# The last chunk's products with w_out as two products of 256 columns each

## The reference, cut to what matters

```
def _moe2_ref(x, w_in, w_out, s, b):
    h = x @ w_in                 # 4608 x 512 @ 512 x 2048
    r = np.maximum(h, 0.0)
    g = s * (r * r) + b
    return (g @ w_out)           # 4608 x 2048 @ 2048 x 512
```

## Time and profile before

| What | us |
| --- | --- |
| median of 3 runs | 681.55 (679.55 to 682.57) |
| the profiled execution's own time | 681.13 |
| its span, first to last instruction | 679.3 |
| PE busy over the span | 646.2 (95%) |
| stretch of the last chunk's products, about 628.0 to 674.7 | 46.7 |

### The profile page before, as it was taken

The page is one execution under the profiler, slowest core; times in us unless marked ns, Lnnn a source line. Parts: engine busy times, 40 slices in busy tenths (PEclk is TensorE's granted clock), DMA queues, the critical chain, the costliest instruction groups (busy, mean ns, idle before and its releaser), DMA issues.

```text
span 679.3 us, 13164 instructions
## 1 busy us (share of the span) xinstructions
PE 646.2 (95%) x5170; PEld 501.3 (74%) x5170; DVE 369.3 (54%) x610; ACT 325.4 (48%) x599; POOL 114.8 (17%) x117
## 2 busy tenths in 40 slices
PE   6787999989998889999999999999999999999997
PEld 6565677767653248888888888888888888888885
DVE  5757575646344747664454454554544554545543
ACT  1576777767421165654344444443444434443442
POOL 3799777622210000000000000000000000000000
PEclk8899999989999999999999999999999999999999
DMA  9688959573489930010010010000000100100101
GB/s 339 223 264 301 357 201 404 172 295 127 156 311 429 425 166 1 1 52 11 1 62 1 1 62 0 25 37 0 31 31 0 62 0 0 62 1 0 63 0 63
DMA packets 25233, 80.45 MB, mean 118 GB/s; under 512 B 6496, under 2 KB 14688, under 8 KB 22368
## 3 DMA queue, kind: packets, MB, share of 16 engines
q1 hardware_dynamic: 25184, 79.76, 31.5%
HBM read 70.32 MB, written 9.44 MB: 117 GB/s over the span
## 4 chain that ended last, share of the span: by engine, by line
PE 83%; DMA 8%; POOL 3%; DVE 2%; issue 2%; ACT 1%; ACTq 0%; SPq 0%; DVEq 0%; POOLq 0%
PE bank L1467 19%; PE bank L1469 19%; PE bank L1468 19%; PE bank L1451 5%; DMA late<-in_moe_w_dram 4%; PE bank L1318 4%; DMA kvbuf<-in_k_dram 3%; PE bank L1305 2%; PE bank L1242 2%; PE bank L1275 2%; PE bank L1401 2%; PE bank L1348 2%; POOL kvbuf L664 1%; PE bank L1364 1%; PE bank L1201 1%
## 5 line engine op out<-in xcount | busy, mean ns | idle before, releaser
L1467 PE MATMUL bank<-w_hi,r_hi 128*128 128x512 f32 x576 | 224.4, 389 | 1.4 <-DVE r_lo L1099 1.4
L1468 PE MATMUL bank<-w_lo,r_hi 128*128 128x512 f32 x576 | 224.2, 389 | 0.0
L1469 PE MATMUL bank<-w_hi,r_lo 128*128 128x512 f32 x576 | 224.2, 389 | 0.0
L1093 DVE SCALAR_TENSOR_TENSOR win_sb<-win_sb,sb_col 128x512 f32<-128x512 f32 x144 | 108.4, 753 | 197.6 <-ACT win_sb L845 197.5
L845 ACT ACTIVATE win_sb<-bank 128x512 f32<-128x512 f32 x144 | 86.2, 598 | 217.7 <-PE bank L1451 217.7
L1467 PEld LDWEIGHTS bank<-w_hi,r_hi 128*128 128x128 f32 x576 | 108.1, 188 | 24.4 <-DVE r_lo L1099 2.0
L1469 PEld LDWEIGHTS bank<-w_hi,r_lo 128*128 128x128 f32 x576 | 108.1, 188 | 22.4
L1468 PEld LDWEIGHTS bank<-w_lo,r_hi 128*128 128x128 f32 x576 | 108.1, 188 | 22.4
L1099 DVE SCALAR_TENSOR_TENSOR r_lo<-win_sb,sb_col,r_hi 128x512 fp32r<-128x512 f32 x144 | 107.6, 747 | 1.5 <-ACT r_hi L854 1.5
L854 ACT ACTIVATE r_hi<-win_sb,sb_col 128x512 fp32r<-128x512 f32 x144 | 103.3, 717 | 1.6 <-PE bank L1469 1.6
L1451 PE MATMUL bank<-cT,g_st 128*128 (+1 forms) x144 | 56.4, 393 | 0.0
(11 more groups left out here) (131 smaller groups left out, 552.3 us busy)
## 6 DMA issues: line engine op xcount, KB each, us to landing
early_third<-in_moe_w_dram SPq DMA_DIRECT2D x6, 2048.0 KB, 14.1
kvbuf<-in_k_dram SPq DMA_DIRECT2D x12, 768.0 KB, 5.5
kvbuf<-in_v_dram SPq DMA_DIRECT2D x12, 768.0 KB, 6.2
out_dram<-win_sb SPq DMA_DIRECT2D x36, 256.0 KB, 2.4
qbuf<-in_q_dram SPq DMA_DIRECT2D x8, 1024.0 KB, 9.1
early<-in_moe_w_dram SPq DMA_DIRECT2D x4, 2048.0 KB, 12.4
late<-in_moe_w_dram SPq DMA_DIRECT2D x4, 2048.0 KB, 20.2
win_sb<-in_moe_w_in_dram SPq DMA_DIRECT2D x4, 1024.0 KB, 5.3
```

Of the source, the lines that this page charges most:

```text
L1093: dve.scalar_tensor_tensor(out=g_sb[:, n % 2, :], in0=r_sb[:, n % 2, :], scalar=sb_col[:, 0:1], in1=r_sb[:, n % 2, :], op0=ALU.mult, op1=A ...
L1467: pe.matmul(acc, r2_hi[:, f % 2, toks], w_hi[:, f, :], start=(f == 0), stop=False)
L1468: pe.matmul(acc, r2_hi[:, f % 2, toks], w_lo[:, f, :], start=False, stop=False)
L1469: last = pe.matmul(acc, r2_lo[:, f % 2, toks], w_hi[:, f, :], start=False, stop=(f == F2C - 1))
```

## The change: what it does

In chunk 8 each product with `w_out` becomes two: the loop over `cols` makes the three products for columns 0 to 255 of the bank and then the three for columns 256 to 511. The weights are loaded anew for each. The flag `start`, which makes a product overwrite instead of add, is set on the first product of the bank alone (f = 0, left half). The two semaphore increments stay on the last product of their m. Chunks 0 to 7 have one part of 512 columns as before.

```
-                        acc = acc_bank(odd, m)[:, :]
-                        pe.matmul(acc, r2_hi[:, f % 2, toks], w_hi[:, f, :], start=(f == 0), stop=False)
-                        pe.matmul(acc, r2_hi[:, f % 2, toks], w_lo[:, f, :], start=False, stop=False)
-                        last = pe.matmul(acc, r2_lo[:, f % 2, toks], w_hi[:, f, :], start=False, stop=(f == F2C - 1))
+                        acc = acc_bank(odd, m)
+                        cols = (slice(0, D // 2), slice(D // 2, D)) if final else (slice(0, D),)
+                        for x, part in enumerate(cols):
+
+                            first_part = f == 0 and x == 0
+                            pe.matmul(acc[:, part], r2_hi[:, f % 2, toks], w_hi[:, f, part], start=first_part, stop=False,
+                                      skip_group_check=True)
+                            pe.matmul(acc[:, part], r2_hi[:, f % 2, toks], w_lo[:, f, part], start=False, stop=False,
+                                      skip_group_check=True)
+                            last = pe.matmul(acc[:, part], r2_lo[:, f % 2, toks], w_hi[:, f, part], start=False, stop=(f == F2C - 1),
+                                             skip_group_check=True)
                         if f == F2C - 1:
                             last.then_inc(acc_ready, 1)
```

## The result

| | us, median | lowest to highest | runs |
| --- | --- | --- | --- |
| before | 679.50 | 676.15 to 685.07 | 20 |
| changed | 683.29 | 679.82 to 686.40 | 20 |

The ratio is 1.0050, with a 95% interval of 1.0029 to 1.0071: 2.0 to 4.8 us more, 3.4 in the middle. The forecast was 682.1 us with a cost of 0.5 us, in a range of 680.3 to 686.5. So the time lies in the range and is slower beyond doubt, but the likeliest case had the cost too small. That 682.1 came within 1.2 us of 683.29 is partly luck: it stood on the three first runs' median of 681.55, which lies 2.05 us above the 679.50 of twenty. On 679.50 the same cost gives 680.0, and 2.6 us would give 682.1.

The account below looks back on a forecast made before the run. PE's pitch in chunk 8 was taken to bound the kernel. Term (3) gave +0.5 us, all else 0, on a median of 681.55 us: 682.1 us, range 680.3 to 686.5.

Parts of the forecast that it names:

- What bounds the kernel: Chunk 8: PE never pauses, DVE and ACT wait for it, so each nanosecond of PE's pitch goes into the end.
- Term (2): Weight loads of chunk 8's 256-column products: pitch at least 111.3 ns, so -0.8 us is the lower end.
- rival of load and extra in line: Chunk 8's products: load of 111.3 ns and 13.3 ns extra add up to 124.6 ns, +4.3 us, 685.9; chance 0.14.
- Term (3): Chunk 8's time above streaming, paid per column or per product: taken mostly per column, pitch 114.1 to 115.0 ns, +0.3 to +0.6 us.
- slower stream: Chunk 8's products: fp32r streams about 5% slower than one column per cycle, so half the columns pay half; +0.3 to +0.6 us.
- per-product part: Chunk 8's products: every fp32r product pays 13.3 ns, pitch 120.0 ns, +2.6 us, 684.1; chance 0.27.
- cheap switches of the fp32 records: Transposes and 512-column fp32 records: 1.6 and 3.3 ns over streaming, taken as the cost of switching products on PE.
- The rule of the Trainium skill that speaks against the change: Chunk 8's loads would not overlap streaming: pitch 218 ns, +40 us; within the unhidden-load or fp32-rate rival, chance 0.06.
- The Trainium skill's N / 2.4 + 2.5 ns: Chunk 8's back-to-back products: 109.2 ns for 256 columns, below the load's floor; 2.5 ns per further product gives +0.5 us.
- (4): Issue of 384 more PE instructions in chunk 8: cost 0, or some tenths of a microsecond if instruction fetch stalled once.
- (5): Waits and neighbours in chunk 8: no wait added or removed, 0.7 us of slack for `r2_lo`; cost 0.
- (6): Tail after the last product, ACT's copies and the stores: cost 0, bounds plus and minus 0.1 us.

Follow-up runs that it names:

- the mixed run: Kernel before, no split, with the two correction products (r2_hi by w_lo, r2_lo by w_hi) taking bf16 operands in all chunks: 679.56 us, ratio 0.9999.

## Why the prediction was right in sign and range, and off in size

- *What bounds the kernel* held: PE at its pitch, nothing else. DVE and ACT only gained slack. The number 682.1 held by luck in part, as said with the result: the cost was 0.5 forecast and 3.4 (2.0 to 4.8) measured, and the base was 2.05 too high.
- *Term (2), the load's floor of 111 ns*, was right; 128-column products run at 111.3. In the rival of load and extra in line, were misread: their 111 ns is the pitch of the loads itself, 4 ns over the streaming and not over the longer of the two.
- *Term (3) is the step that failed.* It took the 13.3 ns of an fp32r product as mostly a slower stream, which gave p = 114.1 to 115.0 and +0.3 to +0.6 us. Measured is 120.0, the value of the rival "per-product part" (chance 0.27): +2.6 us, inside the measured 2.0 to 4.8. Products of 256, 384 and 512 columns have 13.3, 13.5 and 13.3 ns over their columns. The argument for the slower stream, that the record of the last product is as much longer as the pitch, proves nothing about which of the two makes it longer: with one length of product in the trace both readings fit every row. The changed kernel has the second length. Its last record is 282 ns, 106.7 + 175, the same 175 as at 512 columns; that agrees with a part per product, though ends of records are modelled and the pitch is the better witness.

```profile
L1475 PE MATMUL bank<-w_hi,r_lo x1: 282/282/282, 678.5 to 678.5; 128*128 128x256 f32 x1
```

- The cheap switches of the fp32 records were not a guide to fp32r. The run of bf16 halves shows that switches can be as cheap with other operands; for fp32r with whole loads they are not.
- *The rule of the Trainium skill that speaks against the change* ("TensorE: Matmul & The Clock Gate", packing small matmuls: loads overlap only on other rows of the array) does not hold here: at 120.0 ns a load of 111 and a stream of 107 lie side by side. The same section names an exception, a load into the background weight buffer; no run here shows whether that is what happens.
- *The Trainium skill's N / 2.4 + 2.5 ns* ("TensorE: Matmul & The Clock Gate", back-to-back issue gap, given there for a matmul without a budget for its load) gives 109.2 for 256 columns, and the run of bf16 halves has 109.3. For fp32r it falls short by 10.8 ns.
- *Terms (4), (5), (6)*, issue, waits and tail, set at nothing: in chunk 8 PE shows no pause and no wait for `r2_lo`, and from the last product's end to the end of the span it is 4.6 us, as before. Right.
- The rival of load and extra in line (124.6 ns) fell. Its condition was that the array neither streams nor takes a load in the 13.3 ns.

What stays open is what makes the 13.3 ns. Shown is that it doesn't depend on the order of banks or columns, that it changes with the weight columns loaded and the rows written with them (in opposite directions at 256 and 512 columns), and that bf16 products of 256 columns have 2.6 instead. Not shown is the mechanism. A version with all three products in bf16 and 512 columns was not tried; by 10.7 ns for each of 1728 products it might save some 18 us (an estimate from the pitch of 256 columns), at a lower precision of the leading product. The 0.23 us between two bf16 products of 512 columns in the mixed run speaks against counting on it.

## What to carry to other kernels

With fp32r operands and whole loads a product's pitch here is its columns plus a part that is paid again with each product, down to the floor that the load sets; before products are cut up or merged, get that part from two lengths of product in the same operand type, since one length can't tell it from a slower stream. Where the chain is PE from end to end, products should be as wide as the bank allows: halving cost 13 ns for each product cut in two, with nothing to hide it. Compare pitches within one trace rather than total times when an effect is under 1%: the pitch gave the 2.6 us to a tenth, while single runs scatter by 6 us.

## What the runs showed of the hardware that was not expected

- fp32r products with 128 x 128 weights: 13.3 to 13.5 ns over the streaming at 256, 384 and 512 columns, and 111.3 ns at 128, the pitch of the loads.
- Smaller loads, with fewer rows written, made 512-column fp32r products slower: 226.7, 230.0 and 231.7 ns with 128, 64 and 32 weight columns.
- bf16 products of 256 columns: 109.3 ns. But a group of one fp32r and two bf16 products of 512 columns took 0.68 us, what three fp32r products take, and its two bf16 products stood 0.23 us apart.
